# Attention in chunks of 64 tokens on two lanes of partitions, in place of chunks of 96 on one

## What is computed

```python
scores = (1 / sqrt(64)) * q @ k.T                    # 4 batches, 8 heads, 576 tokens, 64 features, float32
Dmat   = gamma[h] ** (i - j) for i >= j, else 0      # gamma[h] = 1 - 2 ** (-5 - h)
x      = (scores * Dmat) @ v                         # retention: attention with decay, no softmax
# x as (2304 tokens, 512), then two feed-forward layers
xn  = x / sqrt(mean(x * x) + 1e-6) * rms_g
y   = (silu(xn @ w_gate) * (xn @ w_val)) @ w_out     # 512 -> 1536 -> 512
h   = y @ w_in                                       # 512 -> 2048
out = where(h >= 1, h, where(h <= -1, 0, (h + 1) ** 2 / 4)) @ w_out2
```

## Time and profile before

| | us |
|---|---|
| median of 3 runs | 912.96 (912.92 to 915.8) |
| the profiled execution, its own time | 914.95 |
| its span, first to last instruction | 913.2 |
| attention: from 0 to the first product of the feed-forward part | 94.66 |
| from there to the end of the span | 818.5 |

### The profile page before, as it was taken

How to read it: one execution, slowest core, us unless ns; L and a number is a source line. 1 busy time by engine, 2 the same in 40 slices (tenths; PEclk the granted TensorE clock), 3 DMA queues, 4 the chain that set the end, 5 groups by cost and what they waited for, 6 DMA issues and landing times.

```text
span 913.2 us, 16544 instructions
## 1 busy us (share of the span) xinstructions
PE 884.4 (97%) x6944; PEld 837.0 (92%) x6944; DVE 471.2 (52%) x606; ACT 435.7 (48%) x688; POOL 261.3 (29%) x179
## 2 busy tenths in 40 slices
PE   6898999999999999999999988999999999999998
PEld 5787999999999999999999988999999888888886
DVE  3497865477954653622243487765657632222220
ACT  2555654445654555512132257877779732222220
POOL 0235764445864664000041321422224200000000
PEclk9998999999999999999999999999999999999999
DMA  9985133333336336334624134242449654444440
GB/s 247 237 240 146 47 99 99 99 98 98 100 98 235 100 98 210 128 105 149 214 74 138 45 136 145 105 150 104 151 161 293 198 155 116 116 115 116 116 125 25
DMA packets 121179, 124.00 MB, mean 136 GB/s; under 512 B 5425, under 2 KB 91569, under 8 KB 121105
## 3 DMA queue, kind: packets, MB, share of 16 engines
q1 hardware_dynamic: 121104, 122.94, 43.2%
HBM read 80.45 MB, written 42.47 MB: 135 GB/s over the span
## 4 chain that ended last, share of the span: by engine, by line
PE 82%; DVE 5%; DMA 5%; ACT 3%; issue 2%; POOL 1%; SPq 1%; ACTq 0%; DVEq 0%
PE pair L614 13%; PE pair L616 13%; PE pair L615 13%; PE pair L746 7%; PE pair L747 7%; PE pair L748 7%; PE pair L712 6%; PE pair L713 6%; PE pair L714 6%; DMA a_kt<-ktok 2%; PE pair L528 1%; DVE cb L1320 1%; PE pair L558 1%; PE pair L564 1%; PE pair L543 1%
## 5 line engine op out<-in xcount | busy, mean ns | idle before, releaser
L614 PE MATMUL pair<-xc,wc 128*128 128x288 f32 x672 | 199.4, 297 | 0.5 <-ACT cp L870 0.2
L615 PE MATMUL pair<-xc,wc 128*128 128x288 f32 x672 | 198.2, 295 | 0.0
L616 PE MATMUL pair<-xc,wc 128*128 128x288 f32 x672 | 197.6, 294 | 0.0
L870 ACT ACTIVATE cp<-pair 128x576 f32<-128x576 f32 x160 | 103.4, 647 | 152.9 <-PE pair L616 147.1
L1408 POOL TENSOR_TENSOR wc<-wt,wc 128x512 fp32r<-128x512 f32 x84 | 122.9, 1486 | 91.9 <-ACT wc L803 77.7
L614 PE MATMUL pair<-xc,wr 128*128 128x288 f32 x448 | 133.9, 299 | 6.9 <-ACT cp L870 6.3
L615 PE MATMUL pair<-xc,wr 128*128 128x288 f32 x448 | 132.2, 295 | 0.0
L616 PE MATMUL pair<-xc,wr 128*128 128x288 f32 x448 | 131.7, 294 | 0.0
L614 PEld LDWEIGHTS pair<-xc,wc 128*128 128x128 f32 x672 | 125.9, 187 | 1.4 <-issue 1.3
L616 PEld LDWEIGHTS pair<-xc,wc 128*128 128x128 f32 x672 | 126.6, 188 | 0.0
L615 PEld LDWEIGHTS pair<-xc,wc 128*128 128x128 f32 x672 | 126.1, 188 | 0.0
(11 more groups left out here) (94 smaller groups left out, 1451.2 us busy)
## 6 DMA issues: line engine op xcount, KB each, us to landing
b_scratch<-cb SPq DMA_DIRECT2D x32, 576.0 KB, 2.9
bv_r<-b_scratch SPq DMA_DIRECT2D x18, 1024.0 KB, 5.8
a_scratch<-cb SPq DMA_DIRECT2D x24, 576.0 KB, 2.9
av_r<-a_scratch SPq DMA_DIRECT2D x8, 1728.0 KB, 8.3
wt<-wB SPq DMA_DIRECT2D x72, 128.0 KB, 2.9
a_k<-kT SPq DMA_DIRECT2D x16, 288.0 KB, 7.9
a_q<-qT SPq DMA_DIRECT2D x16, 288.0 KB, 7.0
a_v<-vtok SPq DMA_DIRECT2D x16, 288.0 KB, 7.8
```

The lines of the kernel that those rows point to most:

```text
L614: pe.matmul(o, wh, xh, start=FIRST[i] and j == 0, stop=False, skip_group_check=True)
L615: pe.matmul(o, wh, xl, start=False, stop=False, skip_group_check=True)
L616: mm = pe.matmul(o, wl, xh, start=False, stop=j == 1, skip_group_check=True)
L870: act.activation(copied(g, n)[:, :, :], pair[(X, Q, X, X)[n]][:, :, 0:HALF], ACT.Copy).then_inc(s_c, 1)
```

## The change

A chunk is 64 tokens, so there are 9. The first eight lie on two lanes: chunks 0 to 3 on partitions 0 to 63, chunks 4 to 7 on partitions 64 to 127 (`NL` is 4). The ninth stands alone on the first lane. A product then has 64 rows, 64 columns and 64 streamed columns. Products of two heads and two lanes go to the four quarters of PE's array, and the two row groups write to different banks. The products of state and q are on the two quarters of the diagonal, ordered so that both row groups use banks of their own, with one wait (`s_in`) ahead of the second half of them. `masked` has one instruction for the eight chunks and one for the ninth. `next_states` has seven steps in place of four. `attended` has two instructions in place of one. Norms in attention are made on 576 columns in two parts of two blocks each, around `next_states`, in place of two halves of tokens under two pairs. SP issues seven DMAs for a pair in place of four. The core of the diff:

```diff
 NB, NH, SEQ, HD = 4, 8, 576, 64
-C = 96
+C = 64
 NC = SEQ // C
...
 
...
                 b, p, i = u // NP, u % NP, u % NK
                 if u >= NK:
-                    sp.wait_ge(s_sc, 2 * (u - NK + 1))
+                    sp.wait_ge(s_sc, u - NK + 1)
                 sp.dma_start(a_k[:, i, :], kT[b, p]).then_inc(d_k[i], 16)
                 if u > 3:
                     sp.wait_ge(s_ob, u - 3)
                 sp.dma_start(a_q[:, p, :, :].rearrange("p c t -> p (c t)"), qT[b, p]).then_inc(d_q[p], 16)
                 if u == 0:
-                    tables(((kdec_s[0:C, :], kdec), (mask_s[0:C, :, :], mask)))
+                    tables((lane, src) for l in range(2) for lane, src in
+                           ((kdec_s[C * l:C * l + C, :], kdec), (mask_s[C * l:C * l + C, :, :], mask)))
                 if u >= NK:
                     sp.wait_ge(s_kd, 2 * (u - NK + 1))
-                sp.dma_start(a_kt[0:C, i, :, :], ktok[b, p]).then_inc(d_kt[i], 16)
-                sp.dma_start(a_v[0:C, p, :, :], vtok[b, p]).then_inc(d_v[p], 16)
+                for l in range(2):
+                    rows, some = slice(C * l, C * l + C), slice(NL * l, NL * l + NL)
+                    sp.dma_start(a_kt[rows, i, :, :], ktok[b, p, :, some, :]).then_inc(d_kt[i], 16)
+                for l in range(2):
+                    rows, some = slice(C * l, C * l + C), slice(NL * l, NL * l + NL)
+                    sp.dma_start(a_v[rows, p, 0:NL, :], vtok[b, p, :, some, :]).then_inc(d_v[p], 16)
+                sp.dma_start(a_v[0:C, p, NL, :], vtok[b, p, :, NC - 1, :]).then_inc(d_v[p], 16)
                 if u == 0:
                     tables(((cdec_s[:, :], cdec), (qdec_s[:, :, :], qdec), (rmsg_s[:, :], rmsg)))
...
-                        pe.wait_ge(s_mask, 2 * (u - 1) + hf + 1)
-                    for c in range(3 * hf, 3 * hf + 3):
+                if u:
+                    pe.wait_ge(s_mask, 2 * u)
+                for j in range(NL + 1):
+                    for l in range(2 if j < NL else 1):
+                        c = l * NL + j if j < NL else NC - 1
                         for h in range(2):
                             rows = slice(HD * h, HD * h + HD)
-                            mm = pe.matmul(b_sc[hf][0:C, h, (c % 3) * C:(c % 3 + 1) * C],
+                            mm = pe.matmul(b_sc[C * l:C * l + C, h, j * C:(j + 1) * C],
                                            a_k[rows, i, c * C:(c + 1) * C], a_q[rows, p, c, :],
                                            start=True, stop=True)
-                    mm.then_inc(s_sc, 1)
+                mm.then_inc(s_sc, 1)
 
             def states(u):
                 b, p, i = u // NP, u % NP, u % 2
                 pe.wait_ge(s_kd, 2 * (u + 1))
...
                 if u:
                     pe.wait_ge(s_st0, u)
                     pe.wait_ge(s_st, (NC - 2) * u)
-                for c in range(NC - 1):
-                    for h in range(2):
-                        rows = slice(HD * h, HD * h + HD)
-                        mm = pe.matmul(b_kv[rows, c * HD:(c + 1) * HD], a_kd[0:C, i, c, rows],
-                                       a_v[0:C, p, c, rows], start=True, stop=True)
+                for j in range(NL):
+                    for l in range(2):
+                        lane = slice(C * l, C * l + C)
+                        for h in range(2):
+                            rows = slice(HD * h, HD * h + HD)
+                            mm = pe.matmul(b_kv[rows, l, j * HD:(j + 1) * HD], a_kd[lane, i, j, rows],
+                                           a_v[lane, p, j, rows], start=True, stop=True)
                 mm.then_inc(s_kv, 1)
 
             def outputs(u):
...
-                        rows = slice(HD * h, HD * h + HD)
-                        pe.matmul(b_ob[rows, c // 3, (c % 3) * C:(c % 3 + 1) * C],
-                                  a_v[0:C, p, c, rows], a_r[0:C, i, c, h, :],
-                                  start=c % 3 == 0, stop=c == 0, skip_group_check=True)
-                for c in range(1, NC):
-                    for h in range(2):
-                        rows = slice(HD * h, HD * h + HD)
-                        mm = pe.matmul(b_ob[rows, c // 3, (c % 3) * C:(c % 3 + 1) * C],
-                                       a_S[rows, i, c - 1, :], a_q[rows, p, c, :],
-                                       start=False, stop=True, skip_group_check=True)
+                    pe.wait_ge(s_ev, 2 * u)
+                for j in range(NL + 1):
+                    for l in range(2 if j < NL else 1):
+                        lane = slice(C * l, C * l + C)
+                        for h in range(2):
+                            rows = slice(HD * h, HD * h + HD)
+                            mm = pe.matmul(b_ob[rows, l, j * C:(j + 1) * C], a_v[lane, p, j, rows],
+                                           a_r[lane, i, j, h, :], start=j == 0, stop=False, skip_group_check=True)
+                mm.then_inc(s_in, 1)
+
+                def from_state(c, h):
+                    rows = slice(HD * h, HD * h + HD)
+                    l, j = (c // NL, c % NL) if c < NC - 1 else (0, NL)
+                    return pe.matmul(b_ob[rows, l, j * C:(j + 1) * C], a_S[rows, i, c - 1, :], a_q[rows, p, c, :],
+                                     start=False, stop=True, skip_group_check=True)
+
+
+                firsts, seconds = (1, 2, 3, NC - 1), (NL, NL + 1, NL + 2, NL + 3)
+                for n in range(NL):
+                    from_state(firsts[n], 0)
+                    from_state(seconds[n], 1)
+                pe.wait_ge(s_in, u + 1)
+                for n in range(NL):
+                    from_state(firsts[n], 1)
+                    mm = from_state(seconds[n], 0)
                 mm.then_inc(s_ob, 1)
 
             def squares(b):
...
                 mm.then_inc(s_ss, 1)
 
-            def spread(b, o, quarters):
+            def spread(b, o):
 
                 pe.wait_ge(s_ri, b + 1)
-                for n, j in enumerate(quarters):
-                    mm = pe.matmul(o[:, n * Q4:(n + 1) * Q4], pick[:, j, :], rinv[b][:, :],
+                for j in range(4):
+                    mm = pe.matmul(o[:, j // 2, j % 2 * Q4:(j % 2 + 1) * Q4], pick[:, j, :], rinv[b][:, :],
                                    start=True, stop=True)
                 mm.then_inc(s_bc, 1)
-
-            def spread_half(b, th):
-                if th:
...
                 if u > 1:
                     act.wait_ge(s_kv, u - 1)
                 for h in range(2):
                     cols = slice(HD * h, HD * h + HD)
-                    act.activation(a_kd[0:C, u % 2, :, cols], a_kt[0:C, i, :, cols], ACT.Copy,
-                                   scale=kdec_s[0:C, 2 * p + h:2 * p + h + 1]).then_inc(s_kd, 1)
+                    act.activation(a_kd[:, u % 2, :, cols], a_kt[:, i, :, cols], ACT.Copy,
+                                   scale=kdec_s[:, 2 * p + h:2 * p + h + 1]).then_inc(s_kd, 1)
 
             def first_state(u):
                 act.wait_ge(s_kv, u + 1)
                 if u > 1:
                     act.wait_ge(s_ob, u - 1)
-                act.activation(a_S[:, u % 2, 0, :], b_kv[:, 0:HD], ACT.Copy).then_inc(s_st0, 1)
+                act.activation(a_S[:, u % 2, 0, :], b_kv[:, 0, 0:HD], ACT.Copy).then_inc(s_st0, 1)
 
             def attended(u):
                 b, p = u // NP, u % NP
                 act.wait_ge(s_ob, u + 1)
-                act.activation(xr[b][:, p, :].rearrange("p (h t) -> p h t", h=2), b_ob[:, :, 0:HALF],
+                act.activation(xr[b][:, p, 0:2 * NL * C].rearrange("p (l t) -> p l t", l=2), b_ob[:, :, 0:NL * C],
                                ACT.Copy).then_inc(s_ev, 1)
+                act.activation(xr[b][:, p, 2 * NL * C:SEQ], b_ob[:, 0, NL * C:(NL + 1) * C], ACT.Copy).then_inc(s_ev, 1)
 
             def square(u):
...
+            dve.wait_ge(d_tab, 112)
 
             def masked(u):
                 p, i = u % NP, u % 2
-                for hf in range(2):
-                    dve.wait_ge(s_sc, 2 * u + hf + 1)
-                    if hf == 0 and u > 1:
-                        dve.wait_ge(s_ob, u - 1)
-                    m = mask_s[0:C, 2 * p:2 * p + 2, :].unsqueeze(1).to_broadcast([C, 3, 2, C])
-                    dve.tensor_tensor(
-                        a_r[0:C, i, 3 * hf:3 * hf + 3, :, :],
-                        b_sc[hf][0:C, :, 0:HALF].rearrange("s h (c t) -> s c h t", c=3), m,
-                        ALU.mult).then_inc(s_mask, 1)
+                dve.wait_ge(s_sc, u + 1)
+                if u > 1:
+                    dve.wait_ge(s_ob, u - 1)
+                dve.tensor_tensor(a_r[:, i, 0:NL, :, :],
+                                  b_sc[:, :, 0:NL * C].rearrange("s h (c t) -> s c h t", c=NL),
+                                  mask_s[:, 2 * p:2 * p + 2, :].unsqueeze(1).to_broadcast([P, NL, 2, C]),
+                                  ALU.mult).then_inc(s_mask, 1)
```

(30 more changed lines are left out.)

61 lines of the change are left out of this document (28 added, 33 removed).

## The result

The changed kernel takes 925.26 us (median of 4 runs, 925.07 to 925.43), the kernel before on the same chip 914.38 us (912.92 to 916.4). The ratio is 1.0117, with a 95% interval of 1.0092 to 1.0142. The forecast was 915.6 us in a range of 907 to 922, with slower as the likeliest of its three cases: the direction came true, the size did not.

The account below looks back on a forecast made before the run. DVE was to bound attention from pair 6: 40.7 start + 0.7 scores + 51.3 DVE + 1.6 outputs + 3.0 late packets put the first feed-forward product at 97.3 for 94.66, +2.6 on 912.96: 915.6 us, range 907 to 922.

Parts of the forecast that it names:

- its three cases: Total time against the kernel before: faster by over 0.3% at 0.27, within 0.3% at 0.27, slower at 0.46.
- PE's work a pair: PE in attention: 44 steps a pair, 2.4 to 3.2 us, taken as 2.8 in place of 3.88.
- the rival of the twos: PE products in attention run two side by side, not four: 4.4 us a pair, total 919 us; chance 8%.
- DVE's work: DVE from pair 6 on: 47.7 us for ten pairs, 4.8 a pair; at 93% busy, 51.3 us.
- the pace passes from PE to DVE: Attention from pair 6 on: DVE's 47.7 us exceeds PE's 34 us for the same ten pairs, so DVE sets the pace.
- Seven issues are 3.0 us a pair, under the pair's 4.8, so SP stays ahead: SP's load queue in attention: seven issues at 0.43 us each stay below DVE's pace, so issuing costs nothing.
- The instruction packets: PE's program fetch in attention: four late packets under full queues; +0.9 us to pair 6, 3.0 us behind it.
- more than eleven: Sign that the forecast is right: more than eleven instruction packets ahead of the first feed-forward product; seventeen forecast.
- more than two: Sign that the forecast is right: more than two PE gaps marked "issue"; four late packets forecast in place of two.
- start and loads: Kernel start and attention loads: table issued later, 0.5 us, and 0.16 MB more bytes, 0.6 us; +1.1 us.
- that rival, at 24%: PE's instructions in attention come in time, DVE 97% busy: first feed-forward product at 90.2 us, total 908.5; chance 24%.
- The clock: PE's clock in attention falls to 1.2 GHz over half the pairs: +6 us on the forecast, 922 us; chance 14%.

Follow-up runs that it names:

- the kernel with four issues and few products: Changed kernel with four load issues a pair for seven and 44 products a pair for 68 from the third pair on, work left out: 909.9 us, ratio 0.9974.
- the kernel with four issues: Changed kernel with k and v by tokens laid out by the host, one DMA each, four issues a pair for seven; all computed: 920.25 us, ratio 1.0076.
- the kernel with seven issues and few products: Changed kernel, seven issues kept, with 44 products a pair in place of 68 from the third pair on, work left out: 918.9 us, ratio 1.0057.
- the kernel before with seven loads: Kernel before with its k and v loads by tokens cut by partitions into two and three DMAs, same bytes, seven issues a pair: 912.11 us, ratio 0.9986.
- the one with few bytes: Kernel before with loads of k and v by tokens carrying only 32 bytes a partition from the fifth pair on, data left out: 908.27 us, ratio 0.9941.
- that with the short chain: Four-issue version of the changed kernel with four of DVE's seven state steps from the third pair on, three left out: 914.92 us, ratio 1.0033.

## Why the prediction missed, step by step

**PE's work a pair: right.** 2.8 us was taken. The chain at the full clock:

```profile
43.07 0.62 PE pair L559 x32
43.70 0.51 PE pair L576 x34
44.21 0.05 PE pair L583
...
44.27 0.87 PE pair L583 x30
45.14 0.67 PE pair L542 x33
```

That is 2.7 us; four products do run side by side, and the rival of the twos is out. PE was busy for 64 to 73% of the windows from 20 to 100 us where 55 to 65% was expected.

**DVE's work: right in size.** A state step takes 278 ns (112 in 31.1 us), the mask 0.69 + 0.27 us. From pair 6's mask to the first product the forecast has 51.3 + 1.6 = 52.9 us without late packets (the 0.7 of the first scores lies ahead of the mask); the kernel with four issues and few products took 88.32 - 34.75 = 53.6. In the changed kernel DVE is busy for 47.9 us from pair 6's mask to the first product, where the forecast had 47.7. But "the pace passes from PE to DVE" is wrong for it: those 62.0 us are 77% and not 93% full.

**"Seven issues are 3.0 us a pair, under the pair's 4.8, so SP stays ahead": this is the step that failed.** The row of 0.43 us was that of a table of 128 rows behind another; five of the seven loads have 64 rows, and with the load behind them five of seven issues take 0.58 to 0.60. Seven are 4.2 us from the first to the next pair's first, and with the long ones among them 4.7 us of issuing in the mean, 4.9 with the 0.04 between them: as long as the pair's 4.8, which leaves nothing to the weights' eight and to a queue that is to run ahead. I had the rate of the pair at hand and asked only if it was smaller than 4.8, not how soon SP would have caught up after each delay. Worth: 5.0 us of the time (four issues against seven; 3.7 by the ratios), 7.1 of the product, half ahead of pair 6 (its mask at 37.41 against 40.88 us) and half behind it. "Perfetto Trace Analysis" of the Trainium skill (What "DMA-bound" means) names an issuing engine's track that is solid DMA slices as a bound of its own; the trace agrees, SP's row of issues is unbroken from 61.57 to 77.84 us.

**The instruction packets: mechanism right, size wrong. This is the second step that failed**, and the reason why the kernel with four issues, in which SP does stay ahead, still takes 920.25 us and not 915.6. 18 packets and five gaps bear out "more than eleven" and "more than two", but I took four late ones at 1.6 us net (0.9 us in the sum ahead of pair 6, 3.0 behind), on the ground that a standing PE drains the queues. The packets are late also with light queues, and every pair asks for 1.08 of them: at 3.8 to 4.25 us a packet that is 4.1 to 4.6 us a pair of supply beside DVE's 4.8. Fewer records gave 6.4 us in the changed kernel (5.5 by the ratios) and 10 with four issues. The Trainium skill ("Runtime: NRT & Kernel Launch", Instruction fetch mechanics) has crossing a block as mostly hidden. The runs contradict it for records of 64 columns: PE stood 18.3 us in eleven such places in the kernel with four issues.

**Where the sum broke.** Pair 0's mask came 0.9 us later than before (10.65, 9.78; I had 1.1 for start and loads, and the table that was to leave 2.2 us later left 4.0 later, at 8.47), pair 6's too (40.88, 40.01), where I had 2.0; from there to the product it is 62.0 us, and the forecast had 51.3 + 1.6 + 3.0 = 55.9. The missing 6.1 us are all behind pair 6's mask, where DVE's sum, SP's issues and the packets meet. I added a fill factor of 93% to DVE's sum, as if DVE had one partner; it had two more that each need nearly the pair's length, and 62.0 us for ten pairs is 6.2 each. The instructions did not come in time (that rival, at 24%, is out for this kernel), but the kernel with four issues and 88 records, which leaves work out, came near it: 909.9 us where it said 908.5.

**The clock.** This rival, 922 us, was nearest in time and is not what was shown. PE did run at the lower level for stretches, 0.51 of 2.4 GHz from 28 to 35 and from 75.9 to 82.8 us, and in the timeline the products with the state then take 1.63 us in place of 1.04. But the kernel with seven issues and few products has 0.83, 0.91, 0.75 and 0.67 in its four windows, less than the changed kernel's 0.83, 0.97, 0.76 and 0.85, and is 6.4 us faster. No run changed the clock by itself, so a share of it stays open.

**Behind the first product** it is 2.0 us more than I held for untouched. But this stretch differs from profile to profile: it is 820.3 us in the kernel before with seven loads and 819.1 in the one with few bytes, where nothing behind attention was changed either, and 818.5 to 822.3 over all the kernels here, so 2.0 us of one profile are no finding. One place where the two differ is the window of 370 to 390 us, in which PE's clock is 0.91 after and 1.00 before:

```profile
370.00:390.00 20.00, 18.09 (x125) 17.89 (x124) 13.32 (x14) 10.37 (x13) 0.00 (x0) 0.91 0.53 176
```

The same dip is in the four-issue kernel and not in that with the short chain. It does not go with the length of the stretch (820.3 us at a clock of 1.00 in the kernel before with seven loads), and why it comes is not settled.

## What to carry to other kernels

Cost the issuing queue like an engine: count its DMAs, price each by a row of the same shape, add the loads of other stages that stand in the same queue, and take it for a rival when the sum, long issues included, comes near the loop. Cutting a product into more and smaller ones that run side by side saves array time but not instructions; in these kernels PE waited for its program where 126 records had less than some 4 us of work. Where several resources come out close to each other, don't multiply one of them by a fill factor: the loop can be longer than the longest, here 6.2 us a pair behind pair 6 where the three needs were 4.9 (SP), 4.1 to 4.6 (instructions) and 4.8 (DVE). And one profile is no measure of a small shift: it placed the end of the stage 4.4 us apart in two kernels of the same time.

## What the runs showed of the hardware

An issue on SP's queue took 0.43 us for 128 or 96 rows and 0.42 for 32, but 0.60 for 64 rows behind 64 rows, whether the source had gaps or not, 0.59 for 128 rows behind 64, and 0.47 for 64 rows behind 128; why stays open. Single issues took up to 2.1 us, and the mean of the changed kernel's was 0.67. On POOL the same load of v took 0.54 us. PE's program came at 126 records in 3.8 us at best (660 records in 20 us, at a DMA share of 0.30) and in 4.25 us at a share of 0.44 to 0.54, and PE went on 1.2 to 1.7 us after the packet that it stood for. No version here that computes everything beats the kernel before: its own variant with seven small loads, at 0.9986 (0.9961 to 1.0012), is not told apart from it.
